# Loading w3's first block and w_out after the first K, and starting the W product one step sooner

## The reference

```python
for t in range(S):                                   # B=4, H=8, S=768, D=48
    kt, vt, rt, wt = k[:, :, t], v[:, :, t], r[:, :, t], w[:, :, t]
    cur = np.einsum('bhd,bhe->bhde', u[None] * kt, vt)
    y[:, :, t] = np.einsum('bhd,bhde->bhe', rt, state + cur)
    state = wt[:, :, :, None] * state + np.einsum('bhd,bhe->bhde', kt, vt)
...
x = y as 3072 x 384
x = ((x @ w1) * (x @ w2)) @ w3 @ w_out               # w1, w2: 384x1024, w3: 1024x1024, w_out: 1024x384
...
P = balanced softmax of x @ w_gate                   # 8 rounds of row and column sums
out = sum over e of P[:, e] * (relu(x @ w1[e]) @ w2[e])   # 8 experts, 1024 wide
```

## Time and profile before

| | us |
|---|---|
| median of 3 runs | 2069.05 |
| lowest and highest | 2068.51 to 2071.92 |
| the profiled execution | 2070.97 |
| its span (first to last instruction) | 2069.2 |
| PE busy in the span | 2018.8 |
| DVE, ACT and POOL busy | 1359.0, 789.0, 611.5 |

### The profile page before, as it was taken

The page is one execution under the profiler, slowest core; times in us unless marked ns, Lnnn a source line. Parts: engine busy times, 40 slices in busy tenths (PEclk is TensorE's granted clock), DMA queues, the critical chain, the costliest instruction groups (busy, mean ns, idle before and its releaser), DMA issues.

```text
span 2069.2 us, 40264 instructions
## 1 busy us (share of the span) xinstructions
PE 2018.8 (98%) x16048; PEld 1673.5 (81%) x16048; DVE 1359.0 (66%) x2129; ACT 789.0 (38%) x1448; POOL 611.5 (30%) x879
## 2 busy tenths in 40 slices
PE   7899999999999999999999999999999999999999
PEld 4699999999777777777868888888877888888887
DVE  4677777773686776777686556665667665566556
ACT  4555555554433333333343333333333333333332
POOL 2376776761564666762020000000020000000000
PEclk9999999999999999999999999999999999999999
DMA  8443343430266677775533444344443445443442
GB/s 214 95 125 108 114 127 102 118 104 20 100 233 212 222 248 242 242 264 197 173 122 128 175 141 164 125 158 141 157 144 114 149 141 175 138 160 133 153 138 97
DMA packets 118585, 316.11 MB, mean 153 GB/s; under 512 B 11920, under 2 KB 45616, under 8 KB 118400
## 3 DMA queue, kind: packets, MB, share of 16 engines
q1 hardware_dynamic: 102768, 259.38, 39.0%
q0 software_dynamic: 14944, 53.68, 7.5%
q10 hardware_dynamic: 688, 0.48, 0.1%
HBM read 239.87 MB, written 71.27 MB: 150 GB/s over the span
## 4 chain that ended last, share of the span: by engine, by line
PE 86%; DVE 7%; issue 3%; ACT 2%; DMA 1%; SPq 0%; POOL 0%; DVEq 0%; ACTq 0%
PE ps L1586 21%; PE ps L1588 21%; PE ps L1587 21%; PE ps L1390 5%; PE ps L1391 4%; PE ps L1392 4%; PE ps L1463 2%; DVE tb L1318 2%; PE ps L1413 2%; ACT h_hi L1019 1%; DVE xs_lo L1093 1%; PE ps L1502 1%; DVE tb L1281 1%; PE ps L1504 1%; DVE h_lo L1286 1%
## 5 line engine op out<-in xcount | busy, mean ns | idle before, releaser
L1019 ACT ACTIVATE h_hi<-tb 128x512 fp32r<-128x512 f32 x378 | 239.0, 632 | 656.9 <-DVE tb L1318 618.7
L1586 PE MATMUL ps<-h_hi,w 128*128 128x512 f32 x1152 | 455.0, 395 | 1.3 <-DVE h_lo L1286 1.1
L1588 PE MATMUL ps<-h_hi,w 128*128 128x512 f32 x1152 | 455.6, 396 | 0.0
L1587 PE MATMUL ps<-h_lo,w 128*128 128x512 f32 x1152 | 454.5, 395 | 0.0
L821 ACT ACTIVATE tb<-ps 128x512 f32<-128x512 f32 x378 | 224.7, 595 | 329.0 <-PE ps L1588 323.7
L1286 DVE SCALAR_TENSOR_TENSOR h_lo<-tb,h_hi 128x512 fp32r<-128x512 f32 x382 | 283.3, 742 | 100.8 <-ACT h_hi L1019 83.8
L1277 DVE TENSOR_TENSOR tb<-tb,ps 128x512 f32<-128x512 f32 x252 | 172.1, 683 | 222.8 <-PE ps L1588 222.6
L1281 DVE TENSOR_TENSOR tb<-ps,tb 128x512 f32<-128x512 f32 x252 | 172.9, 687 | 148.0 <-PE ps L1588 147.9
L1318 DVE SCALAR_TENSOR_TENSOR tb<-tb,Pb 128x512 f32<-128x512 f32 x348 | 255.3, 734 | 18.1
L1586 PEld LDWEIGHTS ps<-h_hi,w 128*128 128x128 f32 x1152 | 216.3, 188 | 54.0 <-issue 3.6
L1587 PEld LDWEIGHTS ps<-h_lo,w 128*128 128x128 f32 x1152 | 217.6, 189 | 50.8
(11 more groups left out here) (159 smaller groups left out, 3298.9 us busy)
## 6 DMA issues: line engine op xcount, KB each, us to landing
early<-w_rows SPq DMA_DIRECT2D x63, 1024.0 KB, 5.5
late<-w_rows SPq DMA_DIRECT2D x63, 896.0 KB, 5.2
w<-w_rows SPq DMA_DIRECT2D x128, 384.0 KB, 4.4
w_rows<-batch POOLq DMA_DIRECT2D x105, 384.0 KB, 3.2
w_rows<-w SPq DMA_DIRECT2D x64, 384.0 KB, 2.7
Pb<-p_rows SPq DMA_DIRECT2D x24, 512.0 KB, 6.2
w_raw<-w POOLq DMA_DIRECT2D x16, 576.0 KB, 5.6
w_raw<-w SPq DMA_DIRECT2D x16, 576.0 KB, 4.8
```

The source lines that it names most:

```text
L1019: nc.scalar.activation(h_hi[:, slot_of(G, b), :], tb[:, t_of(G, b), :], ACT.Relu).then_inc(h_hi_made, 1)
L1586: mm(o, w_hi, x_hi, start=start, stop=False, skip_group_check=True)
L1587: mm(o, w_hi, x_lo, start=False, stop=False, skip_group_check=True)
L1588: return mm(o, w_lo, x_hi, start=False, stop=stop, skip_group_check=True)
```

## The change

W_FROM goes from 3 to 2. The turns of w3 start at step 1 instead of 2 and the products at step 2 instead of 3, and all that follows them on PE, ACT and DVE moves by one step. SP waits for the first K, and no longer for the first decays, before it loads w3's block 0 and w_out. w_out comes in two halves with a semaphore each; `make_W` waits for the first half at m = 0 and for the second at m = 4. Block 1 of w3 is loaded right after the first score, ahead of the next unit's K and R.

```diff
-    W_FROM = 3
+    W_FROM = 2
...
+        wout_loaded = [sem(f"wout_loaded{i}") for i in range(2)]
...
-            sp.wait_ge(w_loaded, PAIR_LOAD)
+            sp.wait_ge(k_loaded[0], PAIR_LOAD)
             load_w3(0)
-            sp.dma_start(wout_raw[:, :, :], moe_w_out.rearrange("(j p) d -> p j d", p=P)).then_inc(wout_loaded, 16)
+            for i in range(2):
+                rows = slice(HB * i, HB * i + HB)
+                sp.dma_start(wout_raw[:, rows, :], moe_w_out.rearrange("(j p) d -> p j d", p=P)[:, rows, :]).then_inc(wout_loaded[i], 16)
             sp.wait_ge(scored, level_no(0, 0))
+            load_w3(1)
             sp.wait_ge(k1_set, 1)
             load_k(1)
             sp.wait_ge(r_set, 2)
             load_r(1)
-            load_w3(1)
...
             def make_W(m):
                 f, j = divmod(m, NF)
-                if m == 0:
-                    pe.wait_ge(wout_loaded, 16)
+                if f == 0 and j % HB == 0:
+                    pe.wait_ge(wout_loaded[j // HB], 16)
```

More of the change, by code:

```diff
@@ L247, in build_program @@
         k_loaded, r_loaded, v_loaded = ([sem(f"{n}_loaded{p}") for p in range(2)] for n in ("k", "r", "v"))
+        wout_loaded = [sem(f"wout_loaded{i}") for i in range(2)]
         wab_loaded = [sem(f"wab_loaded{m}") for m in range(2)]
         w3_loaded = [sem(f"w3_loaded{i}") for i in range(RAW)]
-        w_loaded, u_loaded, consts_loaded, left_loaded, wout_loaded, wg_loaded, first_loaded, p_stored = map(
-            sem, ["w_loaded", "u_loaded", "consts_loaded", "left_loaded", "wout_loaded", "wg_loaded", "first_loaded", "p_stored"])
+        w_loaded, u_loaded, consts_loaded, left_loaded, wg_loaded, first_loaded, p_stored = map(
+            sem, ["w_loaded", "u_loaded", "consts_loaded", "left_loaded", "wg_loaded", "first_loaded", "p_stored"])
         p_loaded = [sem(f"p_loaded{i}") for i in range(2)]
```

## The result

The changed kernel takes 2076.05 us (median of 20 runs, 2070.63 to 2080.05) against 2068.78 (20 runs, 2064.76 to 2073.05) of the kernel before in the same comparison: ratio 1.0035, 95% interval 1.0028 to 1.0041. It is slower by 7.3 us, where 1.7 were forecast, and 1.05 us above the top of the range. The profiled execution has a span of 2077.3 us, 8.1 more than before, and took 2079.19 us, 3.1 above its median, so its parts are not those of a median execution.

A forecast was written before the change was run, and what follows sets the result against it. PE was taken to bound the kernel, busy 2018.8 of 2069.2 us. The terms -2.8 + 2.5 + 1.7 - 0.6 + 0.9 = +1.7 us, added to 2069.05, gave 2070.8 us; range 2065.5 to 2075.0.

The forecast's parts named there:

- The loads of block 0 and w_out: Start of the kernel: block 0 issued at about 6.3 us, 4.7 sooner, w_out right behind; first score unmoved, decays counted 0.
- The landing of block 1: Ahead of the third score: block 1 lands at 18.9 us, fourth score at 23.9 instead of 26.7, minus 2.8 us.
- rival B: Third score: block 1 lands at 21.2 us behind the next K's packets, lower clock follows; 4.0 more, 2074.8 us; chance 0.13.
- the sum of bytes over a rate of 350 GB/s: Startup loads: w_out's data through at about 15 us, block 1's 0.5 MB at 16.4, landing at 18.9 with the tail.
- Block 4 at step 7: Turn at step 7: PE waits 2.5 us for block 4's load, and the lower clock behind it costs another 1.7 us.
- The stop at step 11: Step 11's score: the 2.95 us stop belongs to a place in the code and full DMA queues, and stays; difference 0.
- Rival A: Step 11: the stop vanishes or shrinks as loads after step 7 start sooner, giving back 2.95 + 1.6 us; 2066.2; chance 0.25.
- The end of the startup: Before `go_up(0)`: sixth `wab_lo` 0.6 us sooner against the scores; PE waits about 2.0 and 2.2 us around the last score.
- the half-priced 0.9 us: At `go_up(0)`: lower clock behind the two idle stretches loses up to 1.7 us; half taken, plus 0.9.

## Why the prediction was wrong, step by step

**The loads of block 0 and w_out: right.** Block 0 was issued at 6.26 (6.3 forecast), its turns ran at 12.45 ahead of the second score, and the first and second scores came at 10.87 and 14.29, not late. The decays cost nothing that shows.

**The landing of block 1: the term that had the wrong sign.** Forecast was a landing at 18.9 and the fourth score at 23.9, minus 2.8. The landing came at 21.71 and the lower clock behind it, so the score came at 29.62, plus 2.9. That is 5.7 us of the profiled execution, and its mechanism is rival B's: a landing near the bound of 21.2, the next K's packets, and the clock. B had priced it at 4.0. The step that failed is the sum of bytes over a rate of 350 GB/s. The rate held until 16 us (379), but from 18 to 20 the engines moved 151 GB/s at a share of 1.15: of the 297 packets started then 292 are under 2 KB, mostly those of K, R and the decays behind block 1, and they share the engines with the rest of block 1. The load that was held free of them took 7.1 us. The Trainium skill, "DMA: Bandwidth & Descriptors", section "Queues, rings and completion order", says that each DMA engine takes up a queue's transfers in order, but that a later one may finish before an earlier one. This trace agrees: the first half of K, issued at 12.38 behind block 1, landed after 7.6 us, at 20.0, and block 1 at 21.7. For the lower clock, chance comes in: in five more executions with the same work until 24 us (those with the block 4, `WAB_AT`, filler and w2 edits) the turn of block 1 started at 20.07 to 21.21 after waits of 0.64 to 1.78, the clock stayed at 1.00, and the fourth score came at 25.21 to 26.35, 0.4 to 1.5 us sooner than before. So a usual execution of the change loses less here than its profile, but gains less than the 2.8 of the sum, too.

**Block 4 at step 7: right in kind, too small in price.** The wait was 3.14 us (2.5 forecast), landing 11.4 us after the issue at 39.96. The clock then was low until 58 us and not for one group of products, and took about 3.4 us instead of 1.7. The sum had 4.2, the trace 6.5. Loading block 4 sooner took some 6 us off the median, which confirms the place; the profile behind the change's unaltered front (fillers of steps 14 and 15) had a wait of 2.34 us there and no lower clock. The price of the clock was read from one example and used as a constant: in other executions it cost nothing (behind waits of 1.75 and 2.34 us) or those 1.7 us (ten products of 5.19 behind a wait of 3.02).

**The stop at step 11: the step that was wrong in kind.** "Difference 0" took it for a duration that belongs to a place. It is a meeting of two things: PE's arrival at the end of a block of its instructions, and the q8 packet with the next block, which full DMA queues delay. In four kernels the packet started at 61.52 to 62.22, and PE, which began the score at 60.3 to 61.7, resumed at 64.56 to 65.08 whatever it had gained before. The moment is not fixed: in the five kernels that came later the packet came later too, and PE resumed at 66.30 to 74.57 after shorter stops. The change began the score at 71.1 and lost 0.34; with w2's loads later the stop was not there at all. So it swallowed the gain of the loads alone, and it gave the change back 4.2 us. Rival A had its size right; its reason (loads after step 7 start sooner) was not, since PE came late instead. The Trainium skill, "Runtime: NRT & Kernel Launch", section "Instruction fetch mechanics", which the prediction set against the stop, has the fetch mostly hidden. By the runs the stop is code all the same: under full DMA queues the packet comes too late, and 2.95 to 3.83 us show. The prediction's reading of the earlier trace rows had the wrong packet, that of q14.

**Step 13, which the sum did not have.** Without the stop DVE has no time to catch up: `ruk`, behind a `wab_lo`, starts 1.0 us after the score of step 12 where it started 0.2 after it; it takes 2.97 us instead of 2.13, and PE waits 1.84. It costs 1.3 in the change, and shows as waits of 2.07, 2.25 and 2.07 us in the three kernels in which w2's later loads had removed the stop at step 11 and no other came.

**The end of the startup: right, but for the clock.** The sixth `wab_lo` came 0.6 us sooner against the last score, and both waits are there, 1.86 and 2.23 us (2.0 and 2.2 forecast). Then the half-priced 0.9 us became about 4: the clock was low for all 8 us from 100 to 108. This is the term that fails in the medians too. The fillers took 3 to 4 us off, the earlier parts of w1 and w2 the same against block 4's early load alone. In the fillers' profile `go_up(0)` stood at +0.9, close to the +0.8 to which the sum comes without its clock term, but by luck: block 1, block 4, the stop and the end give -0.6, +2.9, -0.9 and -0.6 there, where the sum has -2.8, +4.2, 0 and -0.6.

**As a whole.** The mechanisms that the prediction named were the ones that acted, in the profiled execution as 5.7 too good at block 1, 2.3 at block 4, 1.3 at step 13, 3.3 at the last clock term, and 4.2 too bad at the stop. With the 1.9 us that came back after the startup that is 6.5, the difference of 8.1 and 1.7 but for rounding. The chance of slower by over 0.2% was given as 0.14 because B and block 4's price were treated as single surcharges; the same cause, PE idle in a moved wait and then slow, stood at three places at once, and the three were not independent. What stays open is why waits of like length are followed by no lower clock in one execution and by 3 to over 8 us of it in another, and how often that happens in the executions of the change that were not profiled.

## What to carry to other kernels

Moving work ahead of a chain moves the transfers that it waits for into that chain: each moved wait needs the landing time of its load with everything that follows it in the queue, not bytes over the peak rate, and the load has to move as far as the work did. A stop marked "issue" in a long row of matmuls can be PE's own instructions coming late: look for the instruction queue's packet that starts 2.7 to 3.0 us before PE goes on. Gains ahead of it are worth little until the loads that delay that packet are spread, and moving those loads can move the stop to the next block. Price an idle stretch of PE of about 2 us or more with its clock behind it, over a range (here 0 to 4 us), not with one example's value.

## What was unexpected of the hardware

- PE's stops marked "issue" ended 2.7 to 3.0 us after the start of a 16 KB packet of the instruction queue q8, at places about 126 matmuls or a multiple of that apart. With w2's loads in the queues such a packet started at 62.22 instead of 56.00.
- A load of 512 KB took 7.1 us to land with the next loads held back, 8.1 to 9.7 with K and R behind it, and 13.5 when it was issued 4.2 us sooner behind w_out.
- Waits of 2.14, 2.23 and 3.14 us brought PE to the lower clock; waits of 1.75, 1.78 and 2.34 us at the first and third of these places in other executions did not; a wait of 2.07 us for DVE at step 13 did in one kernel and not in another, and behind the wait of 2.23 the lower level lasted 8 us in one kernel (100 to 108) and 3 in another (94 to 97).
- Transposes of the identity in the two waits of steps 14 and 15 kept the granted clock at 1.00 behind them in both kernels that had them; in all six profiles that had these waits without fillers the lower level followed.
